# Adding the residual u to the channel sums on VectorE and GpSimd instead of with identity matmuls, in a three-layer fp32 kernel

## The chip, the cores and the metric

The kernel runs on one core of a Trainium2 chip. The metric is the device time of one launch in microseconds (us); where several runs were made, their median counts. TensorE (PE in the profile) multiplies and writes to PSUM; VectorE (DVE), ScalarE (ACT) and GpSimd (POOL) do the elementwise work, and SyncE's queue (SP) issues all the DMAs.

## The reference, cut to what matters

Three layers follow each other, for 4 batches of 768 tokens with 384 channels:

```
attention:  state = f_t * state + k_t v_t^T ;  y_t = q_t state      (8 heads of 48, written in chunks)
layer 2:    h = (x^T @ U @ V)^T ;  u = x + h
            ch = relu(u @ w_ch1) @ w_ch2                            (384 -> 1536 -> 384)
            x2 = u + ch
layer 3:    h = relu(x2 @ w_in)                                     (384 -> 1024)
            out = (h * sigmoid(conv3(h))) @ w_out                   (1024 -> 384)
```

The change concerns the one line `x2 = u + ch`.

## The kernel before, in words

**Split operands.** The matrix products are made from fp32 values in two parts of the type fp32r: a rounded value (hi) and what the rounding left (lo). A product of two such values takes three matmuls: weights hi with data hi, weights lo with data hi, weights hi with data lo. The hi part of a tensor is a cast by ScalarE (`u_hi`, `r_hi`), the lo part a subtraction by VectorE or GpSimd (`u_lo`, `r_lo`).

**Layout.** Layers 2 and 3 work with channels on the partitions and tokens along the free dimension. The 768 tokens of a batch go in two parts (`PARTS`) of 386 and 382 columns. The 384 channels of u are CT = 3 tiles of 128, the 1536 hidden channels of layer 2 are N1 = 12 tiles, the 1024 of layer 3 are N2 = 8.

**Tasks.** `schedule()` (from L65) writes out one list, `ORDER`, and every engine walks that list and does its own share of each task, waiting on semaphores for the others. So a task's place in the list is its place in every engine's queue. For each batch b the list has steps s = 0 to 39:

- `first1` (L593; steps 0 to 23): nine matmuls, L605 to L607, make one tile of `relu(u @ w_ch1)` for one part (q = s; q // 12 is the part). ScalarE then makes `r_hi` (L750), VectorE `r_lo` (L915).
- `second1` (L610; two steps later): nine matmuls, L626 to L628, add that tile's share to the three PSUM banks `acc`, one bank for each tile t of the 384 output channels. For the first tile of a part (j = 0) six matmuls more, L624 and L625, put `u_hi` and `u_lo` into the banks first, through the identity matrix `ident_r`. That is where u is added.
- `x2` after the last tile of a part (steps 13 and 25): ScalarE copies the three banks to `u_hi` in place of u (L756), VectorE subtracts that from the banks to make `u_lo` (L922). The first `second1` of part 1 and the first `second2` wait for `x2_lo_ready`, because they write the banks again.
- `first2` (L631; steps 24 to 39): nine matmuls (L643 to L645) make a tile of `x2 @ w_in`, ScalarE takes the relu (L773), VectorE does three convolution taps (L941, L944), ScalarE the sigmoid (L760), VectorE the product (L928), ScalarE `r_hi` (L766) and GpSimd `r_lo` (L1000). `second2` (L648) follows three steps behind with nine matmuls, L662 to L664.

**Attention in between.** The attention of batch b+1 is woven into the steps of batch b, as three "duos" of 256 tokens with ten stages each. In most steps PE has 64 small matmuls of it, L480 to L542, between `first` and `second`. After stages 0 to 5 (L496), VectorE scales q (L858) and takes scores (L835), and GpSimd scales k (L984); the next stage on PE waits for all three. The last batch has no attention beside it.

**Weights.** During steps 0 to 21 of batch 0 the weights come in as "pieces": SP loads a piece into `conv` or `ostage`, ScalarE rounds it (L729), GpSimd makes the lo part (L994). `ostage` is otherwise the staging tile of the output, and `x` holds the attention's result, which layer 2 reads before its step 0.

Of the kernel before, what the change touches and what calls it, by code (L numbers as in the profile page):

```python
# [64 lines left out]
def schedule():  # L65
# [19 lines left out]
    for b in range(B):  # L85
# [14 lines left out]
        for s in range(2 * N1 + 2 * N2):  # L100
            if s < 2 * N1:
                order.append(("first1", b, s))
                order += [("piece", left.pop(0)) for _ in range(2 if s < 10 else 1) if left]
            else:
                order.append(("first2", b, s - 2 * N1))
            for n, st in at.get(s, []):
                order.append(("att", n, st))
                if st == U and n + 1 < NDUO:
                    order.append(("gates", n + 1))
            q = s - LAG1  # L110
            if 0 <= q < 2 * N1:
                order.append(("second1", b, q))
                if q % N1 == N1 - 1:
                    order.append(("x2", b, q // N1))
            q = s - 2 * N1 - LAG2
            if q >= 0:
                order.append(("second2", b, q))
                if q % N2 == N2 - 1:
                    order.append(("out", b, q // N2))
# [130 lines left out]
def bass_gla_lowrank_mix_ffn_gated_conv_ffn(nc, qT, kT, fT, qn, kn, vn, vp, mix_u, mix_v, w_ch1, w_ch2,  # L250
                                            w_in, conv_w, w_out, mask_in, ident_in, out):
    with ExitStack() as ctx:
# [39 lines left out]
        stages = [conv[:, 0, :], conv[:, 1, :], ostage[:, 0, :], ostage[:, 1, :], ostage[:, 2, :]]  # L292


        with ExitStack() as early:
# [33 lines left out]
        ff1_done, r_hi_ready, r_lo_ready = sem("ff1_done"), sem("r_hi_ready"), sem("r_lo_ready")  # L329
        second_done = sem("second_done")  # L330
        x2_hi_ready, x2_lo_ready = sem("x2_hi_ready"), sem("x2_lo_ready")
        ff2_done, hid_ready, conv_step = sem("ff2_done"), sem("hid_ready"), sem("conv_step")
# [128 lines left out]
        def _(pe):  # L461
# [148 lines left out]
            def second1(b, q):  # L610
                part, j = q // N1, q % N1
                cols, width, s = part_cols(part), PARTS[part][1], slot_of(b, q)
                pe.wait_ge(r_lo_ready, 2 * N1 * b + q + 1)
# [3 lines left out]
                for t in range(CT):  # L617
                    o, ws = acc[:, t, 0:width], slice(t * P, (t + 1) * P)
                    if j == 0:
                        if part == 1:  # L620
                            pe.wait_ge(x2_lo_ready, 2 * CT * b + t + 1)
                        elif b > 0:
                            pe.wait_ge(out_copied, 6 * (b - 1) + 3 + t + 1)
                        pe.matmul(o, ident_r[:], u_hi[:, t, cols], start=True, stop=False)  # L624
                        pe.matmul(o, ident_r[:], u_lo[:, t, cols], start=False, stop=False)  # L625
                    pe.matmul(o, wh[:, j, ws], r_hi[:, s, 0:width], start=False, stop=False)  # L626
                    pe.matmul(o, wl[:, j, ws], r_hi[:, s, 0:width], start=False, stop=False)  # L627
                    mm = pe.matmul(o, wh[:, j, ws], r_lo[:, s, 0:width], start=False, stop=(j == N1 - 1))  # L628
# [19 lines left out]
            def second2(b, q):  # L648
# [6 lines left out]
                for t in range(3):  # L655
                    o, ts = acc[:, t, 0:DM], slice(t * P, (t + 1) * P)
                    if j == 0:
                        if part == 1:
                            pe.wait_ge(out_copied, 6 * b + t + 1)
                        else:  # L660
                            pe.wait_ge(x2_lo_ready, 2 * CT * b + CT + t + 1)
                    pe.matmul(o, r_hi[:, s, ts], wh[:, j, :], start=(j == 0), stop=False)  # L662
# [22 lines left out]
        def _(act):  # L685
# [5 lines left out]
            def attention(n, st):  # L691
# [19 lines left out]
                elif st == Y:  # L711
# [3 lines left out]
                    else:  # L715
                        act.wait_ge(mix_done, 2 * CT * (n // DUOS))
                    heads = x[:, 2 * j:2 * j + 2, :].rearrange("t u (r par e) -> t (u r) par e", par=2, e=D)
                    sums = banks[:, :, 0:EW // 2].rearrange("t par (g e) -> t g par e", e=D)
# [33 lines left out]

            def x2(b, part):
                act.wait_ge(second_done, slots(b, N1 * (part + 1) - 1))
                for t in range(CT):
                    nc.scalar.copy(u_hi[:, t, part_cols(part)], acc[:, t, 0:PARTS[part][1]]).then_inc(x2_hi_ready, 1)  # L756

# [28 lines left out]
            for task in ORDER:  # L786
# [11 lines left out]
                elif kind == "first1":  # L798
                    first1(*task[1:])
                elif kind == "x2":  # L800
                    x2(*task[1:])
                elif kind == "first2":
# [8 lines left out]
        def _(dve):  # L811
# [106 lines left out]

            def x2(b, part):
                for t in range(CT):  # L920
                    dve.wait_ge(x2_hi_ready, 2 * CT * b + CT * part + t + 1)
                    nc.vector.tensor_tensor(u_lo[:, t, part_cols(part)], acc[:, t, 0:PARTS[part][1]],  # L922
                                            u_hi[:, t, part_cols(part)], ALU.subtract).then_inc(x2_lo_ready, 1)

# [41 lines left out]
        def _(pool):  # L966
# [23 lines left out]
            def piece(i):  # L990
# [4 lines left out]
                                        ALU.subtract).then_inc(w_lo_done, 1)  # L995

            def lo2(b, q):
                s = slot_of(b, 2 * N1 + q)
# [4 lines left out]
            for task in ORDER:  # L1003
# [3 lines left out]
                elif kind == "piece":  # L1007
                    piece(task[1])
                elif kind == "first2" and task[2] >= 1:
                    lo2(task[1], task[2] - 1)  # L1010
# [50 lines left out]
```

## Time and profile before

| | before |
|---|---|
| time, median of 3 runs | 752.79 us (752.78 to 753.59) |
| the profiled execution's own time | 753.83 us |
| its span, first to last instruction | 752.0 us |
| mean granted TensorE clock in it | 0.999 of full speed |
| PE busy | 710.0 us, 94% of the span |
| VectorE, ScalarE, GpSimd busy | 58%, 32%, 31% |

How to read the rows: a row of the timeline begins with the start and the duration in us, then the engine, the line of the kernel and what is written and read (with partitions x elements). A bracket at the end says how long the engine sat idle before it and for whom it waited. Matmuls are pipelined: a single one lasts longer than the distance between the starts of two. What a group of matmuls costs is therefore read from starts and not from durations.

### The profile page before, as it was taken

The page shows a single profiled execution, that of the slowest core. Times are in us where ns is not written, and L with a number is a line of the kernel's source. Part 1 is how long each engine was busy: PE and PEld are TensorE (multiplying, and loading weights), DVE is VectorE, ACT ScalarE, POOL GpSimd, SP SyncE. Part 2 cuts the span into 40 slices and gives each one's busy share as a digit, 9 for nine tenths or more (in the row PEclk, how much of TensorE's full clock was granted, in tenths as well). Part 3 has the DMA queues.
Part 4 walks back from the last instruction along what each step waited for, and adds up shares of the span by engine and source line. Part 5 has one row for each costly group of instructions (what it writes and reads, how often), then busy time and mean ns, then how long its engine had stood idle before and what let it go on. Part 6 is the DMA issues. An engine that isn't in the chain of part 4 may idle for free.

```text
span 752.0 us, 23816 instructions
## 1 busy us (share of the span) xinstructions
PE 710.0 (94%) x10784; PEld 668.9 (89%) x10784; DVE 438.5 (58%) x707; ACT 240.8 (32%) x494; POOL 236.5 (31%) x214
## 2 busy tenths in 40 slices
PE   3788789999999989999999999999999999999997
PEld 3676589999999889999999879999999989999997
DVE  6796474473798555354498755363489832121874
ACT  1013624233236322212245431322234541121453
POOL 4674485352343222041233214031044310000232
PEclk9999999999999999999999999999999999999999
DMA  9604343322101110200201200020000000000000
GB/s 190 169 25 116 89 107 90 96 63 48 40 2 54 44 54 10 57 24 23 66 3 35 62 33 24 23 66 23 24 3 1 33 33 1 1 1 1 0 33 32
DMA packets 24292, 33.75 MB, mean 45 GB/s; under 512 B 5152, under 2 KB 17184, under 8 KB 24192
## 3 DMA queue, kind: packets, MB, share of 16 engines
q1 hardware_dynamic: 24192, 32.23, 16.3%
q8 instruction: 85, 1.39, 0.8%
q14 instruction: 15, 0.12, 0.1%
HBM read 27.50 MB, written 4.72 MB: 43 GB/s over the span
## 4 chain that ended last, share of the span: by engine, by line
PE 86%; DVE 6%; issue 3%; POOL 2%; ACT 2%; DMA 1%; SPq 0%; POOLq 0%; ACTq 0%; DVEq 0%
PE acc L626 8%; PE att L496 8%; PE acc L627 7%; PE acc L628 7%; PE hb L605 6%; PE hb L606 6%; PE hb L607 6%; PE acc L662 5%; PE hb L643 5%; PE hb L645 4%; PE hb L644 4%; PE acc L664 4%; PE acc L663 4%; PE att L542 3%; PE hb L576 2%
## 5 line engine op out<-in xcount | busy, mean ns | idle before, releaser
L915 DVE SCALAR_TENSOR_TENSOR r_lo<-hb,r_hi 128x386 fp32r<-128x386 f32 (+1 forms) x96 | 53.5, 557 | 199.7 <-ACT r_hi L750 199.3
L1000 POOL TENSOR_TENSOR r_lo<-conv,r_hi 128x384 fp32r<-128x384 f32 x64 | 61.7, 964 | 242.6 <-ACT r_hi L766 242.6
L750 ACT ACTIVATE r_hi<-hb 128x386 fp32r<-128x386 f32 (+1 forms) x96 | 47.1, 491 | 269.7 <-PE hb L607 269.7
L984 POOL TENSOR_TENSOR k_t<-k_t,blocks 112x512 f32<-112x512 f32 x60 | 81.1, 1354 | 71.9 <-PE att L496 57.1
L626 PE MATMUL acc<-r_hi,w_ch_hi 128*128 128x386 f32 (+1 forms) x288 | 103.0, 358 | 0.0
L605 PE MATMUL hb<-u_hi,w_ch_hi 128*128 128x386 f32 (+1 forms) x288 | 98.6, 342 | 2.2 <-DVE u_lo L909 2.1
L606 PE MATMUL hb<-u_hi,w_ch_lo 128*128 128x386 f32 (+1 forms) x288 | 97.5, 339 | 0.0
L627 PE MATMUL acc<-r_hi,w_ch_lo 128*128 128x386 f32 (+1 forms) x288 | 97.4, 338 | 0.0
L628 PE MATMUL acc<-r_lo,w_ch_hi 128*128 128x386 f32 (+1 forms) x288 | 97.0, 337 | 0.0
L607 PE MATMUL hb<-u_lo,w_ch_hi 128*128 128x386 f32 (+1 forms) x288 | 96.9, 337 | 0.0
L496 PEld LDWEIGHTS att<-q_t,k_t 48*64 48x64 f32 (+3 forms) x3840 | 59.8, 134 | 29.2 <-issue 29.2
L944 DVE SCALAR_TENSOR_TENSOR conv<-hb,convw,conv 128x384 f32<-128x384 f32 x128 | 79.1, 618 | 4.5
L496 PE MATMUL att<-q_t,k_t 48*64 48x32 f32 (+3 forms) x3840 | 66.5, 219 | 14.4 <-DVE scores L829 7.1
L858 DVE TENSOR_TENSOR q_t<-q_t,blocks 112x512 f32<-112x512 f32 x60 | 68.7, 1146 | 10.8 <-PE att L496 6.5
L662 PE MATMUL acc<-w_out_hi,r_hi 128*128 128x384 f32 x192 | 67.8, 353 | 0.6 <-POOL r_lo L1000 0.6
L984 POOL TENSOR_TENSOR k_t<-k_t,gates 112x512 f32<-112x512 f32 x12 | 23.1, 1928 | 142.8 <-PE att L496 142.8
L643 PE MATMUL hb<-u_hi,w_in_hi 128*128 128x388 f32 x192 | 65.5, 341 | 0.0
L645 PE MATMUL hb<-u_lo,w_in_hi 128*128 128x388 f32 x192 | 64.9, 338 | 0.0
L644 PE MATMUL hb<-u_hi,w_in_lo 128*128 128x388 f32 x192 | 64.9, 338 | 0.0
L664 PE MATMUL acc<-w_out_hi,r_lo 128*128 128x384 f32 x192 | 64.8, 338 | 0.0
L663 PE MATMUL acc<-w_out_lo,r_hi 128*128 128x384 f32 x192 | 64.7, 337 | 0.0
L605 PEld LDWEIGHTS hb<-u_hi,w_ch_hi 128*128 128x128 f32 x288 | 54.3, 189 | 3.8 <-DVE u_lo L909 3.5
(128 smaller groups left out, 1289.3 us busy)
## 6 DMA issues: line engine op xcount, KB each, us to landing
q_t<-in_qT_dram SPq DMA_DIRECT2D x24, 192.0 KB, 3.7
k_t<-in_kT_dram SPq DMA_DIRECT2D x24, 192.0 KB, 3.6
gates<-in_fT_dram SPq DMA_DIRECT2D x24, 192.0 KB, 3.8
v_p<-in_vn_dram SPq DMA_DIRECT2D x12, 384.0 KB, 4.1
out_dram<-ostage SPq DMA_DIRECT2D x24, 192.0 KB, 2.0
ostage<-in_w_ch_dram SPq DMA_DIRECT2D x14, 192.0 KB, 3.0
conv<-in_w_ch_dram SPq DMA_DIRECT2D x10, 192.0 KB, 2.5
ostage<-in_w_out_dram SPq DMA_DIRECT2D x5, 192.0 KB, 2.3
```

The source lines that it names most:

```text
L496: mm = pe.matmul(banks[o:o + left, par, g * C:g * C + 32], k[rows, first:first + left], moving, start=True, stop=True, skip_group_check=True)
L605: pe.matmul(o, wh[:, t, ws], u_hi[:, t, cols], start=(t == 0), stop=False)
L606: pe.matmul(o, wl[:, t, ws], u_hi[:, t, cols], start=False, stop=False)
L607: mm = pe.matmul(o, wh[:, t, ws], u_lo[:, t, cols], start=False, stop=(t == CT - 1))
L626: pe.matmul(o, wh[:, j, ws], r_hi[:, s, 0:width], start=False, stop=False)
L627: pe.matmul(o, wl[:, j, ws], r_hi[:, s, 0:width], start=False, stop=False)
L628: mm = pe.matmul(o, wh[:, j, ws], r_lo[:, s, 0:width], start=False, stop=(j == N1 - 1))
L643: pe.matmul(o, wh[:, t, ws], u_hi[:, t, cols], start=(t == 0), stop=False)
L644: pe.matmul(o, wl[:, t, ws], u_hi[:, t, cols], start=False, stop=False)
L645: mm = pe.matmul(o, wh[:, t, ws], u_lo[:, t, cols], start=False, stop=(t == CT - 1))
L662: pe.matmul(o, r_hi[:, s, ts], wh[:, j, :], start=(j == 0), stop=False)
L984: nc.gpsimd.tensor_tensor(view, view, block_product(ends, c, 1), ALU.mult).then_inc(k_ready, 1)
```

## The change

The identity matmuls and the task `x2`'s copies from PSUM go. The banks now hold the channel sums alone. After the last tile of a part:

1. VectorE (`x2`, same place in the list) waits for the last `second1` of the part and adds `u_lo` to each of the three banks, writing an fp32 tile in SBUF (`x2_at`: for part 0 in the rows of `x` that are done with, for part 1 in `ostage`). That frees the bank: `x2_taken`. `second1` of part 1 and the first `second2` wait for this now. For part 1 VectorE also waits for the last weight piece and for the output of the batch before to be stored.
2. GpSimd (`x2_sum`) adds `u_hi` to that tile in place.
3. ScalarE (`x2_split`) rounds the tile to `u_hi`.
4. GpSimd (`x2_split`) subtracts to make `u_lo`.

Steps 2 to 4 are new tasks. For part 0, `x2_sum` of tile t is in step 13 + t and `x2_split` in step 14 + t; for part 1 they are in steps 25 + 2t and 26 + 2t.

```diff
@@ schedule()
+            for part in range(2):
+                i = s - LAG1 - N1 * (part + 1) + 1
+                for t in range(CT):
+                    if i == (part + 1) * t + 1:
+                        order.append(("x2_split", b, part, t))
+                    if i == (part + 1) * t:
+                        order.append(("x2_sum", b, part, t))
@@ buffers
+        def x2_at(part, t):
+            if part == 0:
+                return x[:, 2:UNITS, :].rearrange("p u c -> p (u c)")[:, t * PARTS[0][1]:(t + 1) * PARTS[0][1]]
+            return ostage[:, t, 0:PARTS[1][1]]
@@ tensor: second1
                     if j == 0:
                         if part == 1:
-                            pe.wait_ge(x2_lo_ready, 2 * CT * b + t + 1)
+                            pe.wait_ge(x2_taken, 2 * CT * b + t + 1)
                         elif b > 0:
                             pe.wait_ge(out_copied, 6 * (b - 1) + 3 + t + 1)
-                        pe.matmul(o, ident_r[:], u_hi[:, t, cols], start=True, stop=False)
-                        pe.matmul(o, ident_r[:], u_lo[:, t, cols], start=False, stop=False)
-                    pe.matmul(o, wh[:, j, ws], r_hi[:, s, 0:width], start=False, stop=False)
+                    pe.matmul(o, wh[:, j, ws], r_hi[:, s, 0:width], start=(j == 0), stop=False)
@@ tensor: second2
-                            pe.wait_ge(x2_lo_ready, 2 * CT * b + CT + t + 1)
+                            pe.wait_ge(x2_taken, 2 * CT * b + CT + t + 1)
@@ scalar: attention, stage Y
                         act.wait_ge(mix_done, 2 * CT * (n // DUOS))
+                        if j == 1:
+                            act.wait_ge(x2_lo_ready, 2 * CT * (n // DUOS - 1) + CT)
@@ scalar
-            def x2(b, part):
-                act.wait_ge(second_done, slots(b, N1 * (part + 1) - 1))
-                for t in range(CT):
-                    nc.scalar.copy(u_hi[:, t, part_cols(part)], acc[:, t, 0:PARTS[part][1]]).then_inc(x2_hi_ready, 1)
+            def x2_split(b, part, t):
+                act.wait_ge(x2_ready, 2 * CT * b + CT * part + t + 1)
+                nc.scalar.copy(u_hi[:, t, part_cols(part)], x2_at(part, t)).then_inc(x2_hi_ready, 1)
@@ vector
             def x2(b, part):
+                dve.wait_ge(second_done, slots(b, N1 * (part + 1) - 1))
+                if part == 1:
+                    dve.wait_ge(w_lo_done, len(PIECES))
+                    if b > 0:
+                        dve.wait_ge(stored, 16 * 6 * b)
                 for t in range(CT):
-                    dve.wait_ge(x2_hi_ready, 2 * CT * b + CT * part + t + 1)
-                    nc.vector.tensor_tensor(u_lo[:, t, part_cols(part)], acc[:, t, 0:PARTS[part][1]],
-                                            u_hi[:, t, part_cols(part)], ALU.subtract).then_inc(x2_lo_ready, 1)
+                    nc.vector.tensor_tensor(x2_at(part, t), acc[:, t, 0:PARTS[part][1]],
+                                            u_lo[:, t, part_cols(part)].bitcast(F32), ALU.add).then_inc(x2_taken, 1)
@@ gpsimd
+            def x2_sum(b, part, t):
+                pool.wait_ge(x2_taken, 2 * CT * b + CT * part + t + 1)
+                whole = x2_at(part, t)
+                nc.gpsimd.tensor_tensor(whole, whole, u_hi[:, t, part_cols(part)].bitcast(F32), ALU.add).then_inc(x2_ready, 1)
+
+            def x2_split(b, part, t):
+                pool.wait_ge(x2_hi_ready, 2 * CT * b + CT * part + t + 1)
+                cols = part_cols(part)
+                nc.gpsimd.tensor_tensor(u_lo[:, t, cols], x2_at(part, t), u_hi[:, t, cols],
+                                        ALU.subtract).then_inc(x2_lo_ready, 1)
```

## Rows read from the trace of the kernel before

**Rows 1.** The page: busy time, granted clock, and the chain that ended last.

```profile
PE 710.0 (94%) x10784; PEld 668.9 (89%) x10784; DVE 438.5 (58%) x707; ACT 240.8 (32%) x494; POOL 236.5 (31%) x214
...
PEclk9999999999999999999999999999999999999999
...
PE 86%; DVE 6%; issue 3%; POOL 2%; ACT 2%; DMA 1%; SPq 0%; POOLq 0%; ACTq 0%; DVEq 0%
```

**Rows 2.** The two identity lines by source: count, duration in ns (min/median/max), first and last start.

```profile
L624 PE MATMUL acc<-u_hi,ident_r x24: 332/338/441, 100.5 to 664.0; 128*128 128x386 f32 x12, 128*128 128x382 f32 x12
...
L625 PE MATMUL acc<-u_lo,ident_r x24: 330/340/342, 100.8 to 664.2; 128*128 128x386 f32 x12, 128*128 128x382 f32 x12
```

**Rows 3.** Timeline of PE around the first and the last group of identity matmuls.

```profile
100.50 0.44 PE L624 MATMUL acc<-u_hi,ident_r 128*128 128x386 f32 x1
...
103.26 0.34 PE L605 MATMUL hb<-u_hi,w_ch_hi 128*128 128x386 f32 x1
...
106.02 0.44 PE L626 MATMUL acc<-r_hi,w_ch_hi 128*128 128x386 f32 x1
...
107.69 0.34 PE L605 MATMUL hb<-u_hi,w_ch_hi 128*128 128x386 f32 x1
...
662.29 0.34 PE L624 MATMUL acc<-u_hi,ident_r 128*128 128x382 f32 x1
...
664.92 0.33 PE L605 MATMUL hb<-u_hi,w_ch_hi 128*128 128x382 f32 x1
...
666.48 0.34 PE L626 MATMUL acc<-r_hi,w_ch_hi 128*128 128x382 f32 x1
...
668.05 0.34 PE L605 MATMUL hb<-u_hi,w_ch_hi 128*128 128x382 f32 x1
```

**Rows 4.** Timeline, batch 3, step 13: the old `x2` on ScalarE and VectorE.

```profile
660.91 0.86 ACT L756 CAST u_hi<-acc 128x386 fp32r<-128x386 f32 x2 [1.11 <-PE acc L628]
...
661.43 1.03 DVE L922 TENSOR_TENSOR u_lo<-acc,u_hi 128x386 fp32r<-128x386 f32 x2 [1.03 <-ACT u_hi L756]
```

**Rows 5.** Groups of instructions: total busy us, mean ns of one, idle before and for whom.

```profile
L1000 POOL TENSOR_TENSOR r_lo<-conv,r_hi 128x384 fp32r<-128x384 f32 x64 | 61.7, 964 | 242.6 <-ACT r_hi L766 242.6
...
L766 ACT CAST r_hi<-conv 128x384 fp32r<-128x384 f32 x64 | 32.8, 513 | 35.2 <-DVE conv L928 31.8 <-PE acc L664 3.3
...
L922 DVE TENSOR_TENSOR u_lo<-acc,u_hi 128x386 fp32r<-128x386 f32 x12 | 6.0, 552 | 1.7 <-ACT u_hi L756 1.7
```

**Rows 6.** Timeline: VectorE's scaling of q beside GpSimd's work, and without a GpSimd instruction before it.

```profile
100.29 1.01 POOL L994 TENSOR_TENSOR w_ch_lo<-conv,w_ch_hi 128x384 fp32r<-128x384 f32 x1
...
100.62 2.21 DVE L858 TENSOR_TENSOR q_t<-q_t,blocks 112x512 f32<-112x512 f32 x1 [0.59 <-PE att L496]
101.26 1.02 POOL L994 TENSOR_TENSOR w_ch_lo<-ostage,w_ch_hi 128x384 fp32r<-128x384 f32 x1
102.24 1.76 POOL L984 TENSOR_TENSOR k_t<-k_t,blocks 112x512 f32<-112x512 f32 x1
...
277.04 0.69 DVE L858 TENSOR_TENSOR q_t<-q_t,blocks 112x512 f32<-112x512 f32 x1 [0.52 <-PE att L496]
```

**Rows 7.** Timeline, batch 0, layer 3: GpSimd's `r_lo` of q = 6, and PE's use.

```profile
225.74 1.00 POOL L1000 TENSOR_TENSOR r_lo<-conv,r_hi 128x384 fp32r<-128x384 f32 x1 [2.34 <-ACT r_hi L766]
...
229.32 0.34 PE L662 MATMUL acc<-w_out_hi,r_hi 128*128 128x384 f32 x1
```

**Rows 8.** Timeline, batch 0: scores and k of an attention stage, and PE's next stage.

```profile
102.75 1.31 DVE L835 COPY_PREDICATED scores<-masks,att 128x512 f32<-128x512 uint8 x1
...
104.95 1.14 PE L496 MATMUL att<-q_t,k_t 48*64 48x32 f32 x64
...
164.96 1.53 POOL L984 TENSOR_TENSOR k_t<-k_t,blocks 112x512 f32<-112x512 f32 x1
...
167.09 0.30 PE L496 MATMUL att<-q_t,k_t 48*32 48x32 f32 x12
```

More of the change, by code:

```diff
@@ L330, in bass_gla_lowrank_mix_ffn_gated_conv_ffn @@
         second_done = sem("second_done")
+        x2_taken, x2_ready = sem("x2_taken"), sem("x2_ready")
         x2_hi_ready, x2_lo_ready = sem("x2_hi_ready"), sem("x2_lo_ready")
@@ L611, in second1 @@
                 part, j = q // N1, q % N1
-                cols, width, s = part_cols(part), PARTS[part][1], slot_of(b, q)
+                width, s = PARTS[part][1], slot_of(b, q)
                 pe.wait_ge(r_lo_ready, 2 * N1 * b + q + 1)
@@ L799, in _ @@
                     first1(*task[1:])
-                elif kind == "x2":
-                    x2(*task[1:])
+                elif kind == "x2_split":
+                    x2_split(*task[1:])
                 elif kind == "first2":
@@ L1008, in _ @@
                     piece(task[1])
+                elif kind == "x2_sum":
+                    x2_sum(*task[1:])
+                elif kind == "x2_split":
+                    x2_split(*task[1:])
                 elif kind == "first2" and task[2] >= 1:
```

## The prediction, made before the changed kernel ran

> **What bounds the kernel now.** I read the page first. PE is busy for 94% of the span, at full granted clock in every slice, and the chain that ended last lies on PE for 86% [rows 1]. So a microsecond of matmul that goes is a microsecond of time, wherever nothing else is late just behind it. The source view of the two identity lines gives the amount of work: 24 matmuls each, 48 in all, from 100 us to 664 us [rows 2]. None of their rows has a bracket, so PE never idled in front of them. Then I read the timeline of PE around them, since durations of pipelined matmuls overlap.
>
> **What goes from PE.** In batch 0, step 2, `second1` with its identity matmuls runs from 100.50 to the start of `first1` at 103.26: 2.76 us for 15 matmuls. The next `second1`, with nine, runs from 106.02 to 107.69: 1.67 us [rows 3]. The six cost 1.09 us, some 0.18 each. In batch 3, step 14, it is 662.29 to 664.92 against 666.48 to 668.05: 2.63 less 1.57, 1.06 us [rows 3]. There are eight such groups (two parts, four batches), of which these are the first and the last; the six between give 1.04 to 1.09 by the same reading, and all eight together 8.46 us. Whoever took the median durations instead, 24 x 0.338 and 24 x 0.340 [rows 2], would get 16.3 us; the starts exclude that, since 15 matmuls of 0.34 us took 2.76 us. **Term 1: -8.46 us.**
>
> **What VectorE gets.** Three subtractions from PSUM become three additions from PSUM, of the same shapes, one operand in PSUM and one in SBUF. The nearest row is the old one, 552 ns each [rows 5], or 0.52 each back to back, two in 1.03 [rows 4], and I see no reason for another price, so VectorE's sum stays. They come earlier: before, ScalarE had to copy first, from 660.91, and VectorE followed at 661.43 after 1.03 us idle [rows 4]. Now they start when the last `second1` ends, some 0.5 us sooner, and each frees one bank. PE needs the first bank at 662.29 [rows 3], 1.38 us after 660.91, and the others five matmuls (now three, 0.53 us) later each. Additions ending at about 661.46, 661.97 and 662.5 are in time. This is the tightest place, as no attention lies between. VectorE is blocked from the last `first1` (or `first2`) to that end, with `first1`'s `r_lo` or the next product queued behind; before it was blocked for longer. The two further waits of part 1, in step 25, are for things that the list puts well before it: the last weight piece belongs to step 21, and the outputs of the batch before were staged before this batch's step 0. Cost 0.
>
> **What ScalarE gets.** The same three copies, from SBUF and no longer from PSUM: 513 ns by the cast of the same size in SBUF [rows 5], against 0.43 each back to back [rows 4]. They are spread over three steps and no longer come in one burst, and wait for GpSimd. Queued behind each is the next step's relu, which can start only when PE has finished that step's nine matmuls, 1.57 us or more [rows 3]. ScalarE is busy for 32% [rows 1]. Cost 0, but with no cover if GpSimd is late by a step.
>
> **What GpSimd gets.** Two operations per tile, 48 in all. The nearest row is its subtraction of 384 columns, 964 ns [rows 5]; the weight pieces of the same width take 1.01 to 1.02 [rows 6]. That is 46 to 49 us more on an engine with 236.5 us busy [rows 1]. What waits for it: `first2` needs `u_lo` of part 0 in step 24, made by step 16 or 17, and of part 1 in step 32, made in step 30, with a whole step between (3.13 us or more, 664.92 to 668.05) [rows 3]. What queues behind it: the scaling of k for the attention, which PE waits for, and in layer 3 `r_lo` for `second2`. Batches 1 and 2, layer 2: in a step GpSimd has one scaling of k, 1.5 us [rows 8], and now two operations, 3.5 of 4.4 us (103.26 to 107.69) [rows 3], and the new ones come after the scaling. Cost 0. Batch 0, steps 14 to 17, adds a weight piece of 1.0 us ahead of the scaling: 1.0 + 1.5 + 2.0 = 4.5 against 4.4 us per step, less where the attention's stage is shorter; I allow a backlog of 0.3 in each of two steps. The k of stage 4 is ready at 164.96 + 1.53 = 166.49 and PE uses it at 167.09, a reserve of 0.6 us [rows 8]; the backlog of twice 0.3 uses it up. I take 0.1, bounds 0 to 0.6 (the whole backlog with no reserve).
>
> **What becomes late next on PE.** Where a group shrinks by 1.05 us, the next attention stage comes 1.05 us sooner. In batch 0, step 2, scores are taken until 102.75 + 1.31 = 104.06, and PE would be there at 104.95 - 1.09 = 103.86 [rows 8]: it waits 0.2 to 0.3 us. The stage after it waited for GpSimd already, so part of this is no new loss. I take 0.1, bounds 0 to 0.3. At the other five groups with attention beside them the reserve is over 1 us, and in batch 3 there is none to wait for.
>
> **The port.** VectorE's scaling of q has both inputs in SBUF. It takes 0.69 us when nothing of GpSimd runs before it, and took 2.21 us when it came to two GpSimd subtractions, until the second had ended [rows 6]. So each new GpSimd operation may hold such an instruction for about 1 us. In layer 2 VectorE has room. In layer 3 of batches 0 to 2 it is nearly full, and there three scalings of q fall beside the three `x2_split` of part 1. PE's reserve there is the time from `r_lo` to its use: 225.74 + 1.00 = 226.74 to 229.32, 2.58 us [rows 7], the smallest of the nine I followed. Three holds of 0.5 (the split gets in behind the scaling and hits only the small product after it) stay inside. I take 0, bounds 0 to 1.3 (three holds of 1 us are 3.0, less 2.58 is 0.4 per batch, times three). The Trainium skill speaks against the change here: "SBUF — State Buffer", section "Who interferes with whom", says that the read port pair is an exclusive lock between a VectorE instruction with two SBUF inputs and a GpSimd one that reads SBUF, with the later one fully blocked. By that rule, the trace agrees (the 2.21 us), and the additions from PSUM, with one SBUF input, would be free of it; it would leave the sum between my value and the upper bound.
>
> **The sum.** -8.46 + 0.1 + 0.1 = -8.3 us, against the profiled execution's own 753.83: 745.5. That execution was 1.04 us above the median of the three runs, 752.79, so by the median it is **744.5 us**. A change of 0.2%, 1.5 us, is about what can be told from none here.
>
> **Rivals.**
> 1. *GpSimd or the port shows through* in layer 3 or in batch 0: for it, a VectorE that hardly idles in layer 3; against it, the 2.58 us reserve. All upper bounds together: 0.6 + 0.3 + 1.3 = 2.2 us lost, 746.5; about 745.2 to 747. Chance 0.17.
> 2. *The gain is given back at the attention.* A wait for scores or k takes the matmuls' place in the six groups that have attention beside them, and only batch 3 keeps its 2.1 us: 750.7. For it, the 0.2 us of rows 8; against it, the reserves elsewhere. Chance 0.03.
> 3. *Slower: VectorE falls behind in layer 3.* If all six new operations of part 1 hold VectorE for their whole 1 us, it is 6 us late, 6 - 2.58 = 3.4 more than PE's reserve, in three batches: +10.3, so 752.8 - 8.5 + 10.3 = 754.6. It decides from 5.4 us of holds per batch (2.58 + 8.46 / 3). Against it: three of the six (`x2_sum`) lie in steps without a scaling of q. Chance 0.03.
> 4. *The removed work was not on the path*, or a hand-over through three engines stalls each part by 1.06 us: 752.8. The tight place above has 0.8 us in hand before the first bank is late. Chance 0.02.
>
> **How the numbers follow.** The forecast, 743.8 to 745.2, has the rest, 0.75. Its low end is 8.46 with no cost and 0.5 for the spread of runs (752.78 to 753.59). The range of 8 in 10 reaches into the first rival: 743.8 to 746.8. Faster by over 0.2%: the forecast, rivals 1 and 2, 0.95. Rival 4 is the 0.02 for the same, rival 3 the 0.03 for slower.
>
> **What would show it.** Right: the eight first `second1` of a part take 1.57 to 1.7 us; 48 matmuls fewer; PE busy some 8 us less while its idle time, about 42 us, stays; no row of PE waiting for the new additions; GpSimd near 284 us busy; the new additions near 0.55 us. Wrong: PE idle at `second1` of step 14 for VectorE's additions, at `second2` for `r_lo` L1000's successor in steps 26 to 32, or at attention stages 2 to 5 for scores or k; ScalarE waiting for `x2_sum` long enough to delay a relu. The forecast falls if the distance between starts in the nine that remain grows, as the first write of a bank would then have been dearer than I took it.

## The result, and the profile after

| | before | after |
|---|---|---|
| time, median of 5 runs | 753.59 us (752.78 to 755.16) | 747.90 us (747.04 to 749.11) |
| the profiled execution's own time | 753.83 us | 747.90 us |
| its span | 752.0 us | 746.1 us |
| PE busy | 710.0 us | 704.2 us |
| GpSimd busy | 236.5 us | 287.1 us |
| first `second1` to last matmul in the trace | 647.31 us | 640.90 us |

The ratio of the times is 0.9923, 95% interval 0.9903 to 0.9943: 5.7 us faster, where 8.3 were forecast. The time lies above the range, which ended at 746.8.

The last line of the table needs a word, because the argument below rests on it. Up to the first `second1` all kernels here run the same instructions, and yet this stretch took 100.50 us before, and 100.96, 101.04 and 101.30 in three traces of the changed kernel; over all traces it ranges from 99.90 to 103.31. What comes after it repeats: to the start of the last matmul it is 747.81 - 100.50 = 647.31 us before, 741.86 - 100.96 = 640.90 after, and 640.96 and 640.90 us in the two other traces of the changed kernel. In none of the 14 traces does the granted clock fall in it. So kernels are compared below by the distance from the first `second1` to the last matmul, which I call the **path**, and by the timed medians beside it.

The page of the changed kernel, busy time and the chain that ended last:

```profile
PE 704.2 (94%) x10736; PEld 662.0 (89%) x10736; DVE 441.0 (59%) x707; ACT 241.7 (32%) x494; POOL 287.1 (38%) x262
...
PE 78%; DVE 10%; issue 4%; POOL 3%; ACT 2%; DMA 1%; SPq 0%; POOLq 0%; ACTq 0%; DVEq 0%
```

48 matmuls fewer, 48 GpSimd instructions more. Against [rows 1], the chain lies on PE for 78% and no longer for 86%, and on VectorE for 10% and no longer for 6%. That shift is a first hint that VectorE's work reaches PE somewhere where it did not before; the experiments have to show where.

Timeline of PE, the first group of batch 0 and the one after it, to be laid beside [rows 3]:

```profile
100.96 0.44 PE L639 MATMUL acc<-r_hi,w_ch_hi 128*128 128x386 f32 x1
...
102.66 0.34 PE L620 MATMUL hb<-u_hi,w_ch_hi 128*128 128x386 f32 x1
...
105.49 0.45 PE L639 MATMUL acc<-r_hi,w_ch_hi 128*128 128x386 f32 x1
...
107.18 0.34 PE L620 MATMUL hb<-u_hi,w_ch_hi 128*128 128x386 f32 x1
```

The group that took 2.76 us takes 102.66 - 100.96 = 1.70, as the next one does (1.69). I laid the starts of all groups of matmuls of the two traces side by side. In each of the eight places the changed kernel gains 1.04 to 1.08 us, 8.48 in all. It loses 0.68, 0.59 and 0.55 us again at one place in each of batches 0, 1 and 2, and 0.1 us here and there elsewhere. This is that place in batch 0, the first `first2` of part 1 (step 32), on PE and on GpSimd:

```profile
222.93 0.33 PE L658 MATMUL hb<-u_lo,w_in_hi 128*128 128x388 f32 x1
223.68 0.45 PE L656 MATMUL hb<-u_hi,w_in_hi 128*128 128x388 f32 x1 [0.41 <-POOL u_lo L1024]
...
220.16 1.02 POOL L1030 TENSOR_TENSOR r_lo<-conv,r_hi 128x384 fp32r<-128x384 f32 x1 [1.14 <-ACT r_hi L780]
221.13 1.08 POOL L1003 TENSOR_TENSOR k_t<-k_t,blocks 112x512 f32<-112x512 f32 x1
222.17 1.46 POOL L1024 TENSOR_TENSOR u_lo<-ostage,u_hi 128x382 fp32r<-128x382 f32 x1
```

PE waits for the `u_lo` of the third tile, the `x2_split` of step 30. GpSimd comes to it late: the scaling of k ahead of it (L1003) starts at 221.13, though PE had started that attention stage at 216.35. Between them stands `r_lo` (L1030), which waits for ScalarE and, through it, for VectorE's convolution.

VectorE at the attention stage of step 26, before and after (`q`, scores, and the small product of gates; after, with GpSimd's split beside it):

```profile
207.62 1.43 DVE L858 TENSOR_TENSOR q_t<-q_t,blocks 112x512 f32<-112x512 f32 x1
208.97 0.69 DVE L835 COPY_PREDICATED scores<-masks,att 128x512 f32<-128x512 uint8 x1
209.57 0.28 DVE L865 TENSOR_TENSOR blocks<-blocks 112x128 f32<-112x128 f32 x1
```

```profile
205.98 1.42 DVE L872 TENSOR_TENSOR q_t<-q_t,blocks 112x512 f32<-112x512 f32 x1
207.33 0.70 DVE L849 COPY_PREDICATED scores<-masks,att 128x512 f32<-128x512 uint8 x1
207.93 0.50 DVE L879 TENSOR_TENSOR blocks<-blocks 112x128 f32<-112x128 f32 x1
...
206.81 1.46 POOL L1024 TENSOR_TENSOR u_lo<-ostage,u_hi 128x382 fp32r<-128x382 f32 x1
```

The small product (two inputs in SBUF) takes 0.50 us where it took 0.28; the two others are as they were. It comes while GpSimd's new `x2_split` runs (206.81 to 208.27 us). The same 0.22 us is lost in steps 28 and 30.

To see what VectorE's chain does as a whole, I took the start of the product with the gate (L928 before, L947 after) of tile 0 and of tile 12 of a batch's layer 3. Batch 0, before and after:

```profile
201.61 0.58 DVE L928 TENSOR_TENSOR conv<-hb,conv 128x384 f32<-128x384 f32 x1
...
245.10 0.55 DVE L928 TENSOR_TENSOR conv<-hb,conv 128x384 f32<-128x384 f32 x1
```

```profile
199.97 0.58 DVE L947 TENSOR_TENSOR conv<-hb,conv 128x384 f32<-128x384 f32 x1
...
244.14 0.55 DVE L947 TENSOR_TENSOR conv<-hb,conv 128x384 f32<-128x384 f32 x1
```

43.49 us before, 44.17 after: 0.68 longer, as much as PE lost in that batch. It might be asked which of the two delays the other. Between these two products VectorE is idle for 5.05 us before and 5.06 after, 4.0 of it in the same six waits for ScalarE's sigmoid and the rest in gaps of at most 0.1 us. No gap there is put down to PE, so the 0.68 us do not come from PE's wait. This idle sum is 5.05 or 5.06 us in batch 0 of every run below.

### The profile page after: what moved, and what is told of

It reads as the page before. It is cut to its first block, busy times and chain, and to the rows that moved or that the text cites. A ratio compares the mean times of both kernels' runs of the same rounds, so it can differ in the third digit from the quotient of the medians.

```text
span 746.1 us, 23772 instructions
## 1 busy us (share of the span) xinstructions
PE 704.2 (94%) x10736; PEld 662.0 (89%) x10736; DVE 441.0 (59%) x707; ACT 241.7 (32%) x494; POOL 287.1 (38%) x262
## 4 chain that ended last, share of the span: by engine, by line
PE 78%; DVE 10%; issue 4%; POOL 3%; ACT 2%; DMA 1%; SPq 0%; POOLq 0%; ACTq 0%; DVEq 0%
PE acc L639 8%; PE att L511 7%; PE hb L620 7%; PE acc L640 7%; PE acc L641 6%; PE hb L621 6%; PE hb L622 6%; PE acc L675 4%; PE att L557 3%; PE acc L677 3%; PE acc L676 3%; PE hb L656 3%; PE hb L658 3%; PE hb L657 3%; PE hb L591 2%
## 5 line engine op out<-in xcount | busy, mean ns | idle before, releaser
L1030 POOL TENSOR_TENSOR r_lo<-conv,r_hi 128x384 fp32r<-128x384 f32 x64 | 61.7, 964 | 154.6 <-ACT r_hi L780 154.6
L1003 POOL TENSOR_TENSOR k_t<-k_t,blocks 112x512 f32<-112x512 f32 x60 | 81.5, 1361 | 54.6 <-PE att L511 41.2
L1003 POOL TENSOR_TENSOR k_t<-k_t,gates 112x512 f32<-112x512 f32 x12 | 23.7, 1972 | 142.7 <-PE att L511 142.6
```

What stands on the lines that cost most here:

```text
L1003: nc.gpsimd.tensor_tensor(view, view, block_product(ends, c, 1), ALU.mult).then_inc(k_ready, 1)
```

## The experiments

Each was timed in five rounds beside the kernel before on its chip: r1 to r4 on one, r5 to r8 on another, r9 to r12 on a third. The kernel before had a median of 755.03, 755.03 and 755.02 us there; the ratios go by these, and the first two rows of the table are the pair of the section above. "Path" and "gate 0 to 12" (the distance just described, in batch 0) come from one trace of each run.

| run | median, us | ratio to before (95%) | path, us | gate 0 to 12, us |
|---|---|---|---|---|
| before | 753.59 | | 647.31 | 43.49 |
| after | 747.90 | 0.9923 (0.9903 to 0.9943) | 640.90 | 44.17 |
| r1 after again | 748.27 | 0.9907 (0.9894 to 0.9920) | 640.96 | 44.18 |
| r12 after, third | 749.46 | 0.9929 (0.9903 to 0.9954) | 640.90 | 44.18 |
| r3 wasted identity matmuls | 756.85 | 1.0026 (1.0008 to 1.0043) | 649.35 | 44.18 |
| r4 no u added | 746.85 | 0.9890 (0.9877 to 0.9903) | 639.01 | 43.52 |
| r7 part 0 only | 750.25 | 0.9934 (0.9918 to 0.9950) | 643.28 | 43.52 |
| r2 dense part 1 | 749.57 | 0.9924 (0.9911 to 0.9937) | 642.20 | 44.89 |
| r6 last split ahead | 747.92 | 0.9902 (0.9886 to 0.9918) | 641.07 | 44.18 |
| r8 split on VectorE | 750.36 | 0.9932 (0.9912 to 0.9952) | 643.20 | 44.91 |
| r5 odd steps | 746.74 | 0.9899 (0.9879 to 0.9920) | 639.10 | 43.52 |
| r11 odd steps again | 746.23 | 0.9885 (0.9863 to 0.9907) | 638.96 | 43.51 |
| r9 output copies ahead | 748.07 | 0.9905 (0.9885 to 0.9926) | 638.89 | 44.15 |
| r10 delay on VectorE | 746.27 | 0.9888 (0.9861 to 0.9915) | 639.70 | 43.74 |

### What the matmuls are worth: r1, r3, r4, r7

**r1** is the changed kernel, unchanged.

> The changed kernel once more, beside before on one chip. The theory of three terms (-8.46 us of matmuls; +1.8 us from PE waiting for the last u_lo of part 1 in step 32 of batches 0 to 2; +0.9 us from a stretch of half TensorE clock near 97 to 100 us): about 5.8 us under before, with the half-clock stretch and the three waits in the trace again. The rival for the clock term, chance: the stretch is absent, and the time is about 6.7 us under before.

Measured: 748.27 us, ratio 0.9907, against 755.03 for before on this chip, 6.8 us under it, as the rival for the clock term had it. The three waits in step 32 are there again (0.70, 0.58, 0.53). PE's start distances near 97 us were normal in this trace. In the first trace of the changed kernel they were not:

```profile
97.49 0.52 PE L620 MATMUL hb<-u_hi,w_ch_hi 128*128 128x386 f32 x1
97.81 0.52 PE L621 MATMUL hb<-u_hi,w_ch_lo 128*128 128x386 f32 x1
```

0.32 us from start to start, not 0.18, at a granted clock of 0.50 from 97 to 99 us, that is 1.2 GHz. In r1 lower clocks lie between 70 and 90 us, in r5 between 80 and 90. Yet the first `second1` came at 100.96 us in the trace with the stretch at 97 us and at 101.04 in r1, so these traces don't bear out the term of 0.9 us. Such stretches wander in the weight-loading stretch from run to run, ahead of the first changed instruction, and are no effect of the change.

**r3** puts the 48 identity matmuls back as waste.

```diff
+                    if j == 0:
+                        pe.matmul(o, ident_r[:], u_hi[:, t, part_cols(part)], start=True, stop=False)
+                        pe.matmul(o, ident_r[:], u_lo[:, t, part_cols(part)], start=False, stop=True)
                     pe.matmul(o, wh[:, j, ws], r_hi[:, s, 0:width], start=(j == 0), stop=False)
```

> The changed kernel with the 48 identity matmuls put back as pure waste: they write the banks and the first real matmul overwrites them. If the matmuls are worth their distance between starts and lie on the path in all eight places: 8.4 us slower than the changed kernel, about 2.7 us slower than before (1.8 of waits in step 32 and, if it returns, 0.9 of half clock). If some of the gain had been given back at the attention: less than 8 us over the changed kernel.

Measured: the path is 8.45 us longer than the changed kernel's (649.35 against 640.90), and the median 8.6 us above r1. Nothing of it was given back at the attention. Against before the path is 2.04 us longer, the median 1.8 us: that is the price of the whole new way of adding u, without its gain.

**r4** takes the matmuls out of the kernel before and puts nothing in their place: it leaves out the addition of u.

```diff
# the kernel before, second1
-                        pe.matmul(o, ident_r[:], u_hi[:, t, cols], start=True, stop=False)
-                        pe.matmul(o, ident_r[:], u_lo[:, t, cols], start=False, stop=False)
-                    pe.matmul(o, wh[:, j, ws], r_hi[:, s, 0:width], start=False, stop=False)
+                    pe.matmul(o, wh[:, j, ws], r_hi[:, s, 0:width], start=(j == 0), stop=False)
```

> The kernel before without its 48 identity matmuls: u is not added at all, x2 is the channel sums alone, and nothing is put in VectorE's or GpSimd's queue. This is term 1 by itself: 8.4 us under before, that is 2.6 us under the changed kernel, if no half-clock stretch appears, or 7.5 us if it does. The rival, that the additions elsewhere cost nothing and the missing part lies in the matmuls being worth less: 5.8 us under before, equal to the changed kernel.

Measured: ratio 0.9890, the median 8.2 us under before (755.03), the path 8.30 us shorter. The matmuls are worth their starts. This is what the change could bring at most, and the changed kernel's path is 1.89 us short of it, not 2.6, as the half-clock stretch is not the change's.

**r7** makes half of the change: part 0 as in the changed kernel, part 1 as before.

```diff
# schedule: x2_sum and x2_split for part 0 only; the old x2 on ScalarE and VectorE for part 1
-            for part in range(2):
+            for part in range(1):
# tensor: second1
+                        if part == 1:
+                            pe.matmul(o, ident_r[:], u_hi[:, t, cols], start=True, stop=False)
+                            pe.matmul(o, ident_r[:], u_lo[:, t, cols], start=False, stop=False)
```

> One half of the change: part 0 is added by VectorE and GpSimd, part 1 still by identity matmuls and the old x2. If part 0's work is hidden whole: 4.2 us under before (24 matmuls), no wait in step 32, so that part 1 of the change brings 4.2 less 1.8, and this kernel is 2.4 us slower than the changed one. If part 0 costs something too (batch 0 with its weight pieces): the rows of GpSimd and PE in steps 13 to 17 of batch 0 show it, and it is less than 4.2 us under before.

Measured: path 4.03 us shorter than before. The four groups of step 2 gave 4.24, and small drifts took 0.2, as they did in r4 (8.30 of 8.46). Its path is 2.38 us longer than the changed kernel's, where 2.4 were expected. Steps 13 to 17 show no shift against before in any batch, batch 0 with its weight pieces included, and the gate distance stays at 43.52. Part 0 is hidden. The loss lies in part 1, in layer 3.

### Where the 1.9 us go: r2, r6, r8

My first theory was a matter of place: the last split stands behind the scaling of k, in a queue that is late. Three kernels tried it.

**r2** puts part 1's operations one step apart.

```diff
-                    if i == (part + 1) * t + 1:
+                    if i == t + 1:
                         order.append(("x2_split", b, part, t))
-                    if i == (part + 1) * t:
+                    if i == t:
                         order.append(("x2_sum", b, part, t))
```

> x2_sum and x2_split of part 1 one step apart, as in part 0 (sums in steps 25, 26, 27, splits in 26, 27, 28), nothing else changed. If the wait in step 32 comes from GpSimd's last split standing too late in its queue: PE's wait for u_lo in step 32 is gone in all three batches, 1.8 us faster than the changed kernel. If it comes from the port between VectorE and GpSimd and only moves: the same work now falls in steps 26 to 28, PE waits there for r_lo or k by a like amount, and the time stays within 0.5 us of the changed kernel.

Measured: the wait for `u_lo` is gone, and yet the path is 1.30 us longer than the changed kernel's. Neither expectation held; the second named the right direction, but not the size. GpSimd and VectorE in step 26 of batch 0:

```profile
206.34 1.17 POOL L1003 TENSOR_TENSOR k_t<-k_t,blocks 112x512 f32<-112x512 f32 x1
207.47 1.01 POOL L1024 TENSOR_TENSOR u_lo<-ostage,u_hi 128x382 fp32r<-128x382 f32 x1
208.43 1.45 POOL L1019 TENSOR_TENSOR ostage<-ostage,u_hi 128x382 f32<-128x382 f32 x1
...
206.62 2.40 DVE L872 TENSOR_TENSOR q_t<-q_t,blocks 112x512 f32<-112x512 f32 x1
```

VectorE's scaling of q takes 2.40 us. It ends at 209.02, 0.54 us after the second of three GpSimd operations that follow each other without a gap (208.48), and alone it takes 0.69; so nearly all of its work was done after that second one had ended, as in [rows 6]. In the changed kernel it took 1.42. PE then waits at the next attention stages and, in step 35, at the first `second2` of part 1: 0.26 + 0.23 + 0.24 + 0.67 = 1.40 us in batch 0. The gate distance grew by 44.89 - 43.49 = 1.40 as well. Batch 1 is alike (gate distance 1.44 longer), but in batch 2 it grew by only 0.45, and PE lost 0.43 at that place.

**r6** moves one operation of the changed kernel.

```diff
+            if s == 30:
+                order.append(("x2_split", b, 1, 2))
             for n, st in at.get(s, []):
                 order.append(("att", n, st))
```

> The changed kernel, with only the last x2_split of part 1 moved: in step 30 it comes ahead of the attention's scaling of k, not behind it. If PE's wait in step 32 is a matter of that place in GpSimd's queue: the split ends 1.4 us earlier, before PE needs it, and the kernel is 1.2 to 1.8 us faster than the changed one. If it is the port: the split and the scaling of k still have to share it with VectorE's scaling of q, k or q comes 1 us later, and PE waits at the attention stage of step 32 instead; no gain, within 0.4 us.

Measured: path 641.07, no gain. The split ends in time, and no attention stage waits either. PE meets the same loss three steps later, at the first `second2` of part 1: 0.69, 0.74 and 0.67 us in the three batches. Batch 0:

```profile
235.39 0.41 PE L677 MATMUL acc<-w_out_hi,r_hi 128*128 128x384 f32 x1 [0.54 <-POOL r_lo L1032]
```

In batch 1 the profile names ScalarE's output copy L800 for it. In batch 0 it names `r_lo`, but the `r_lo` of this tile had ended at 232.28 us, three microseconds before. What ended last was the first output copy, at 234.77 + 0.48 = 235.25:

```profile
234.07 0.80 ACT L724 COPY k_end<-att 128x768 f32<-128x768 f32 x1
234.77 0.48 ACT L800 COPY ostage<-acc 128x384 f32<-128x384 f32 x1
```

The gate distance is unchanged, 44.18. So the place in the queue was a symptom. VectorE's chain is 0.68 us late, and whichever of its dependents comes first stops PE.

**r8** gives the splits of part 1 to VectorE.

```diff
# gpsimd: x2_split
+                if part == 1:
+                    return
# vector: x2_split, new, for part 1 only, at the same place in the list
+                dve.wait_ge(x2_hi_ready, 2 * CT * b + CT * part + t + 1)
+                nc.vector.tensor_tensor(u_lo[:, t, cols], x2_at(part, t), u_hi[:, t, cols],
+                                        ALU.subtract).then_inc(x2_lo_ready, 1)
```

> The changed kernel, with the three x2_split of part 1 (u_lo) taken from GpSimd and given to VectorE, 0.5 to 0.6 us each with both inputs in SBUF, at the same places in the list. My prediction held that VectorE is nearly full in layer 3: then its chain slips by about 0.6 us per tile, 1.8 us per batch, inside the 2.6 us that PE has in hand, and as u_lo is no longer behind the scaling of k, the wait in step 32 goes: 1 to 1.8 us faster than the changed kernel. If VectorE has no such reserve: PE waits for r_lo or scores in steps 28 to 36, and it is slower than the changed kernel.

Measured: path 2.30 us longer than the changed kernel's. The gate distance grew by 44.91 - 43.49 = 1.42 us, three subtractions of some 0.47 each in the chain, and PE lost 1.48, 1.39 and 1.34 us. It lost them in step 32, waiting for `u_lo`; I had expected a wait for `r_lo` or scores:

```profile
224.56 0.44 PE L656 MATMUL hb<-u_hi,w_in_hi 128*128 128x388 f32 x1 [1.21 <-DVE u_lo L949]
```

VectorE has no 2.6 us to give away: this `u_lo` had no such reserve either.

### Where VectorE's lateness meets PE: r5, r11, r10, r9

**r5** keeps GpSimd's new work of part 1 away from VectorE's two-input instructions: nothing of it in a step with an attention stage.

```diff
+                sums, rounds, splits = [((0, 1, 2), (1, 2, 3), (1, 2, 3)), ((0, 0, 2), (1, 2, 3), (2, 4, 4))][part]
                 for t in range(CT):
-                    if i == (part + 1) * t + 1:
+                    if i == rounds[t]:
+                        order.append(("x2_hi", b, part, t))      # ScalarE
+                    if i == splits[t]:
                         order.append(("x2_split", b, part, t))   # GpSimd
-                    if i == (part + 1) * t:
+                    if i == sums[t]:
                         order.append(("x2_sum", b, part, t))
```

> GpSimd's six operations of part 1 are put in steps without an attention stage: sums of tiles 0 and 1 in step 25, sum of 2 and split of 0 in step 27, splits of 1 and 2 in step 29 (ScalarE rounds in steps 26, 27, 28). If the loss in layer 3 has the two sources seen so far, the last split standing behind the scaling of k (the changed kernel) and VectorE's scaling of q held by GpSimd operations queued behind the scaling of k (the dense version), both are gone: no wait of PE for u_lo in step 32, none for scores, 1.8 us faster than the changed kernel, level with the kernel that adds no u. If GpSimd's added work delays r_lo or k by its mere amount, wherever it stands: within 0.5 us of the changed kernel.

Measured: 746.74 us, ratio 0.9899; path 639.10, 1.80 us shorter than the changed kernel's and level with r4, which adds no u at all (639.01). The gate distance is back at 43.52. GpSimd does the same 48 new operations. The small product of step 26 is back at 0.28 us:

```profile
206.91 0.28 DVE L881 TENSOR_TENSOR blocks<-blocks 112x128 f32<-112x128 f32 x1
```

**r11** is r5 once more, and **r12** the changed kernel, on one chip.

> The kernel of r5 again, on the same chip as the changed kernel, for the timed difference: 1.8 to 2.0 us faster than the changed kernel.

> The changed kernel again, beside r11: the same three losses of 0.55 to 0.7 us at step 32; 6 to 7 us under before. The first 90 us vary by a microsecond from run to run, in before as well.

Measured: 746.23 (744.66 to 748.03) against 749.46 us (746.67 to 750.99); paths 638.96 and 640.90. The medians are 3.2 us apart, more than the 1.94 of the paths. The intervals of the ratios, 0.9863 to 0.9907 and 0.9903 to 0.9954, just touch. Over the two pairs of timed runs (r5 and r1 were on two chips) the gain is seen each time, and its size is best taken from the paths. In r12 the losses in step 32 were 0.70, 0.58 and 0.54 us.

**r10** delays VectorE in r5 without any GpSimd in it.

```diff
# vector: attention, third duo of a batch beside layer 3
+                    if n >= DUOS and j == 2 and st in (2, 3, 4):
+                        nc.vector.memset(idle[:], 0.0)
```

> The kernel of r5 (odd steps, no waits left), with a memset of 128x128 on VectorE into a tile that nobody reads, in attention stages 2, 3 and 4 of the third duo (steps 26, 28, 30): some 0.2 us each, and no GpSimd in it. If VectorE paces layer 3 of batches 0 to 2 with 0.1 us in hand: each batch is longer by the three delays less 0.1, that is 0.5 us for 0.2 each, seen at the first second2 of part 1 (step 35), 1.5 us in all. If PE has the 2.58 us in hand that my prediction took: no change.

Timeline of VectorE, step 26 of batch 0:

```profile
208.29 0.17 DVE L881 MEMSET idle<- 128x128 f32 x1
208.38 0.22 DVE L884 TENSOR_TENSOR blocks<-blocks 112x128 f32<-112x128 f32 x1
```

The memset lasts 0.17 us, but pipelined with its neighbours it delays the chain by less: the gate distance grew by 43.74 - 43.52 = 0.22 us for three. PE lost 0.25, 0.26 and 0.23 us in the three batches, each at the first `second2` of part 1, where I expected it; the path grew by 0.60 to 0.74 us against the two traces of r5. The size of 1.5 us did not hold, because the delays were 0.07 and not 0.2 us; the rule did: PE loses what VectorE loses, all of it. The reserve is nil. This rests on the traces: the timed medians (746.27 here, 746.74 and 746.23 for r5 and r11) spread too much to show 0.7 us.

**r9** asks where PE meets VectorE. In ScalarE's queue of step 34 it puts the output copies of part 0 ahead of the copy of `k_end`, on top of r6.

```diff
# scalar
+            mine = list(ORDER)
+            for b in range(B - 1):
+                turn, copies = mine.index(("att", DUOS * (b + 1) + 2, T)), mine.index(("out", b, 0))
+                mine[turn], mine[copies] = mine[copies], mine[turn]
-            for task in ORDER:
+            for task in mine:
```

> The kernel of r6 (last split ahead of the scaling of k), with one thing more: in ScalarE's queue of step 34 the three output copies of part 0 stand ahead of the copy of k_end (0.80 us), not behind it. Theory now: VectorE is held 3 x 0.22 = 0.66 us per batch by GpSimd's splits, and what PE meets first is not r_lo (2.58 us in hand) but the output copies, which stand in ScalarE's queue behind VectorE's chain with 0.1 us in hand. Moved ahead they have 0.9 us in hand: the waits of 0.7 us at the first second2 of part 1 go, in all three batches, though VectorE stays 0.66 us late; some 2 us faster than r6. Rival, that VectorE's lateness reaches PE by another way just as soon (r_lo, free banks of the ring): the same loss appears at another place in steps 32 to 39, no gain.

Measured: path 638.89, 2.18 us shorter than r6. The waits at the first `second2` of part 1 are gone in all three batches, though VectorE is as late as in r6 (44.15). The lateness used up what the move gave: the first copy ended some 0.16 us before PE wrote the bank.

```profile
236.14 0.47 ACT L800 COPY ostage<-acc 128x384 f32<-128x384 f32 x1
...
236.78 0.40 PE L677 MATMUL acc<-w_out_hi,r_hi 128*128 128x384 f32 x1
```

The median, 748.07, does not show it. In the profiled execution the first `second1` came at 102.94 us, 2.1 us later than in r6; for the other executions there is no trace, and on its chip r9 is 1.4 us under r12 and 1.8 above r11. By the path of one trace, r9 is level with r5. So the output copies were the tight point. With them moved, VectorE's 0.65 us cost PE nothing. The rows of the kernel before show how tight it was:

```profile
235.14 0.80 ACT L709 COPY k_end<-att 128x768 f32<-128x768 f32 x1
...
235.83 0.48 ACT L784 COPY ostage<-acc 128x384 f32<-128x384 f32 x1
...
236.46 0.41 PE L662 MATMUL acc<-w_out_hi,r_hi 128*128 128x384 f32 x1
```

The first output copy ends at 236.31, and PE writes that bank again at 236.46. These 0.15 us are no reserve: where PE did stand idle for this copy the distance is the same, 0.14 us in r6 (235.25 to 235.39) and in r2, 0.15 in r10. It is the hand-over from ScalarE to PE. The matmul ahead of it started at 236.27, so PE lost 0.01 us here against the usual 0.18, and 0.08 in batch 1 (411.92 to 412.18). In the kernel before, nothing was in hand at this point. The copy stands in ScalarE's queue behind the casts and sigmoids, and these follow VectorE's chain.

## Why the prediction was wrong, point by point

**Direction and main term: right.** Eight groups of six matmuls at 1.06 us, -8.46 us. Removed alone they are worth 8.30 (r4), put back 8.45 (r3). Reading starts and not durations was what counted: by durations it would have been 16.3.

**VectorE's and ScalarE's prices: right.** The additions took 547 ns in part 1 and 556 in part 0, in the mean, against 552 forecast, the copies from SBUF 508 and 509 against 513. The tight place that I had named, step 14 of batch 3, was in time.

**GpSimd: the price was nearly right (busy 236.5 to 287.1 us, where 284 were forecast; the splits of part 1 took 1.35 us in the mean and not 1.0), the cover was not.** My text said of the `u_lo` of part 1: "made in step 30, with a whole step between". A step of the list is a place in each engine's queue and not a time. GpSimd came to step 30's attention stage at 221.13, 4.8 us after PE had started it, so the whole step between was used up before it began. I had the row that shows this lag, [rows 7] with `r_lo` of q = 6 at 225.74, and read only its distance to its own consumer.

**Batch 0, layer 2: sizes small, as predicted.** At the attention stage after the first `second1` PE waited for scores (0.33 us in r1), and got it back at the next stage; that stage is in step 3, and not in step 2 as the prediction has it. The backlog of GpSimd in steps 14 to 17 cost nothing on PE (I had 0.1).

**The port: the mechanism was right, the reserve wrong. This is the step that failed.** The text had it: "Three holds of 0.5 (the split gets in behind the scaling and hits only the small product after it) stay inside." This happens, at 0.22 us each and not 0.5, three times per batch. What failed is "PE's reserve there is the time from `r_lo` to its use: 225.74 + 1.00 = 226.74 to 229.32, 2.58 us". That is the reserve of one dependent of VectorE's chain. Another, the output copies in ScalarE's in-order queue, had none (the 0.15 us of the rows above is the hand-over), and in the changed kernel the late `u_lo` met PE still earlier. I had followed nine tiles of `r_lo` and not looked at what else stands behind VectorE. With the right reserve the term would have been 3 x 0.68 = 2.0 us, and the sum -6.3, near the 6.41 us by which the path shrank. The rival "GpSimd or the port shows through", to which I gave 0.17, is what came: the path lost 8.46 - 6.41 = 2.05 us where it allowed 2.2, though the time, 747.90, lies above its 747. I had also set an upper bound of 1.3 us for this term, with the same wrong reserve in it, so the range ended too low.

The rule of the Trainium skill that I weighed ("SBUF — State Buffer", "Who interferes with whom": the read port pair is an exclusive lock between a two-input VectorE instruction and a GpSimd one that reads SBUF) agrees with these traces: 2.40 us for a scaling behind two GpSimd operations, 0.50 instead of 0.28 for the small product, and no change for the additions, which have one input in PSUM.

**The rest.** Path -6.41, start stretch +0.46, together -5.95 in the profiled pair, against -5.93 in their own times. The start stretch lies ahead of the first changed instruction. My median came from runs at 752.79; the five runs put before at 753.59. So of the 3.4 us between 744.5 and 747.9, 1.89 are the path (8.30 forecast, 6.41 measured), 0.80 the median of before, 0.46 the start, and 0.25 the scatter between the profiled pair and the medians.

One sign did not serve: PE was to be busy some 8 us less at an idle time of about 42. It was busy 5.8 us less and idle for 41.9, and the three waits can't be read from that. In r5, whose path is level with r4's, PE was busy for 705.1 and idle for 38.1 us; in r4 it was 702.8 and 41.6. These sums hold the start stretch too, and say less than the distances between starts.

Not tried: r9's order of ScalarE's queue together with r5's steps. By the paths r5 is level with the kernel that adds no u, so I would expect nothing from it.

## What to carry to other kernels

Before calling an engine's delay covered, follow every consumer behind it, through the in-order queues of other engines too, and take the smallest reserve. Before calling a distance between two engines a reserve, look at the same distance where the second one is known to have waited: what is left there is hand-over. And look at how busy an engine is in the stage itself: VectorE was idle for 5.05 of 43.49 us in layer 3, never for PE, while the page gives it 58% of the span. Place names in a hand-written order are not times: read how far each engine lags behind the busiest one before putting work "a whole step" ahead of its use. And when GpSimd gets work that reads SBUF, put it where VectorE runs instructions with one SBUF input; the same amount of work then cost nothing.

## What the runs showed that I had not expected

A wait removed on PE may only move. In the changed kernel and in r6 the waits are for different tiles in different steps, and the loss is the same 0.7 us per batch, since it is VectorE's lateness that is paid. The start distance over a dozen periods of the pacing engine, 43.5 us here, measured this to 0.03 us in batch 0, when the timed medians spread over a microsecond or more. In batch 1 it has two values for the same kernel, 43.66 us in r5 and 44.04 in r11; where it is longer, VectorE has an additional wait of 0.28 us for ScalarE near its start. So one batch alone does not do.

Two VectorE instructions of the same kind fared differently at GpSimd's hands. A scaling of q that came to GpSimd operations queued without a gap was passed over between two of them (2.40 us in r2, 2.21 in [rows 6]), while in the changed kernel it got in behind the first (1.42), and the split after it waited (1.46 instead of 1.01 us). Which of the two happens I can't say from these traces.

Stretches of TensorE at 1.2 GHz lie between 60 and 102 us, where weights come in, in 11 of the 14 traces, at varying places and whatever the kernel. The arrival at the first `second1` spreads over 3.4 us (99.90 to 103.31), and the clock alone does not explain it: r3, with four such stretches, has the latest arrival, but r4 and r8 have none and arrive at 101.21 and 101.02, and r5, with one, at 99.90. What else spreads it these runs don't show.
